# The perceptron's first products as pairs of 64 rows, with relu and window shared out, and stage 1 begun with its r chunks

## The reference

```python
h_mlp = np.maximum(pos_emb @ w1, 0.0) @ w2           # pos_emb 12480x64, w1 64x64, w2 64x128
h_filt = h_mlp * np.exp(-0.01 * pos)[:, None]
u = x * v
y = np.fft.irfft(np.fft.rfft(u, n=2*S, axis=1) * np.fft.rfft(h_filt, n=2*S, axis=0)[None], n=2*S, axis=1)[:, :S]
x1 = x * y                                           # 12480x128
x2 = np.maximum(x1 @ w_in, 0.0)**2 @ w_out           # 128 -> 2048 -> 128
h2 = x2 @ w_in2
out = (np.maximum(h2, 0.0) + alpha * np.minimum(h2, 0.0)) @ w_out2
```

## Time and profile before

| | us |
|---|---|
| median of 3 runs | 1376.6 (1376.57 to 1376.84) |
| profiled execution, its own time | 1377.39 |
| profiled execution, span of the engines' records | 1375.4 |
| TensorE busy | 1367.1 (99%) |
| VectorE busy | 1117.0 (81%) |
| ScalarE busy | 1124.1 (82%) |
| GpSimd busy | 178.9 (13%) |

### The profile page before, as it was taken

One profiled execution on the slowest core, in us unless ns is written; L12 is line 12 of the kernel. 1 busy time (PEld: TensorE's weight loads), 2 busy tenths in 40 slices (PEclk: granted clock), 3 DMA queues, 4 the chain that ended last, 5 costly groups with the idle time before them and its releaser, 6 DMA issues.

```text
span 1375.4 us, 19834 instructions
## 1 busy us (share of the span) xinstructions
PE 1367.1 (99%) x6879; PEld 1153.8 (84%) x6879; DVE 1117.0 (81%) x1398; ACT 1124.1 (82%) x1505; POOL 178.9 (13%) x200
## 2 busy tenths in 40 slices
PE   9999999999999999999999999999999999999998
PEld 8988888998888888888888888888888888888887
DVE  6888888568778877887888888887888878888888
ACT  3678888358878877888888888888888888888887
POOL 4647888410000000000000000000000000000000
PEclk9999999999999999999999999999999999999999
DMA  9648896620000100000000000000000000000000
GB/s 258 186 123 254 276 286 216 198 71 28 24 32 8 32 24 9 8 1 8 8 8 8 1 8 8 8 8 1 8 8 8 0 8 9 8 8 0 8 9 15
DMA packets 53514, 75.34 MB, mean 55 GB/s; under 512 B 5285, under 2 KB 37515, under 8 KB 53435
## 3 DMA queue, kind: packets, MB, share of 16 engines
q1 hardware_dynamic: 52507, 73.58, 17.3%
q10 hardware_dynamic: 832, 0.47, 0.1%
q0 software_dynamic: 96, 0.20, 0.1%
HBM read 54.93 MB, written 19.23 MB: 54 GB/s over the span
## 4 chain that ended last, share of the span: by engine, by line
PE 97%; ACT 1%; DVE 1%; issue 0%; DMA 0%; POOL 0%; SPq 0%; ACTq 0%; DVEq 0%; POOLq 0%
PE ps L190 13%; PE ps L192 13%; PE ps L191 13%; PE ps L205 13%; PE ps L207 13%; PE ps L206 13%; PE ps L783 5%; PE ps L820 4%; PE ps L904 3%; PE ps L798 3%; PE ps L806 2%; PE ps L791 1%; PE ps L766 1%; DVE stage L400 1%; PE ps L871 0%
## 5 line engine op out<-in xcount | busy, mean ns | idle before, releaser
L414 DVE TENSOR_TENSOR g_lo<-stage,g_hi 128x1024 fp32r<-128x1024 f32 (+2 forms) x199 | 238.2, 1198 | 164.3 <-ACT g_hi L315 163.7
L190 PE MATMUL ps<-x_hi,w_hi 128*128 128x512 f32 (+2 forms) x800 | 310.3, 388 | 0.2 <-DVE x_lo L390 0.2
L205 PE MATMUL ps<-g_hi,w_hi 128*128 128x512 f32 (+2 forms) x800 | 308.8, 386 | 0.6 <-DVE g_lo L414 0.4
L192 PE MATMUL ps<-x_lo,w_hi 128*128 128x512 f32 (+2 forms) x800 | 307.5, 384 | 0.0
L191 PE MATMUL ps<-x_hi,w_lo 128*128 128x512 f32 (+2 forms) x800 | 307.3, 384 | 0.0
L207 PE MATMUL ps<-g_lo,w_hi 128*128 128x512 f32 (+2 forms) x800 | 307.2, 384 | 0.0
L206 PE MATMUL ps<-g_hi,w_lo 128*128 128x512 f32 (+2 forms) x800 | 307.2, 384 | 0.0
L324 ACT ACTIVATE relu<-ps 128x1024 f32<-128x1024 f32 (+2 forms) x200 | 201.6, 1008 | 107.2 <-PE ps L192 104.6
L400 DVE SCALAR_TENSOR_TENSOR stage<-stage,alpha_sb 128x512 f32<-128x512 f32 (+2 forms) x400 | 276.4, 733 | 0.4 <-ACT stage L357 0.2
L357 ACT ACTIVATE stage<-ps,sign_sb 128x512 f32<-128x512 f32 (+2 forms) x400 | 251.2, 673 | 2.7 <-PE ps L192 1.4
L446 DVE TENSOR_TENSOR g_lo<-g,g_hi 128x1024 fp32r<-128x1024 f32 (+2 forms) x200 | 239.3, 1196 | 13.1 <-ACT g_hi L345 13.0
(11 more groups left out here) (68 smaller groups left out, 1213.5 us busy)
## 6 DMA issues: line engine op xcount, KB each, us to landing
g_dram<-work SPq DMA_DIRECT2D x49, 256.0 KB, 3.4
work<-dft_back SPq DMA_DIRECT2D x66, 128.0 KB, 3.6
gt<-g_dram SPq DMA_DIRECT2D x10, 784.0 KB
gt<-x_seq SPq DMA_DIRECT2D x32, 196.0 KB
work<-v_seq SPq DMA_DIRECT2D x32, 196.0 KB
work<-dft_forward SPq DMA_DIRECT2D x49, 128.0 KB, 3.5
x<-x_gate SPq DMA_DIRECT2D x16, 390.0 KB, 4.9
out_t<-x SPq DMA_DIRECT2D x23, 256.0 KB, 2.0
```

The costliest lines, as they stand in the source:

```text
L190: nc.tensor.matmul(into[:, c, :t], w_hi[k][:, at], x_hi[layer][:, :t], start=True, stop=False)
L192: last = nc.tensor.matmul(into[:, c, :t], w_hi[k][:, at], x_lo[layer][:, :t], start=False, stop=True)
L205: nc.tensor.matmul(acc[layer][:, :t], w_hi[k][:, at], hi[:, c], start=first, stop=False)
L414: nc.vector.tensor_tensor(lo[:, :, :t], g2[at][:, :, :t], hi[:, :, :t].bitcast(FP32), ALU.subtract).then_inc(g2_lo_ready, 1)
```

## The change

Three things are changed together. First, each of the 64 products becomes two of 64 rows (`HALF[half]`), one for each block, at `tile_position` (0, 0) and (64, 0), into two different banks; the moving side is one 64x64 square of w1. The weights are 128 columns of `pos_sb` instead of 98, so that 30 columns of the next residue are multiplied too, into rows of PSUM that nobody reads (the very last residue takes 98). A product therefore waits for the piece that holds the next residue. Second, of fills 1, 3 and 5 block 1 goes another way: ScalarE applies the relu and writes `h_sb`, and GpSimd multiplies this by the window, before its first x * v. Third, stage 1 begins with two r chunks, which wait for all of h, and the order of chunks is another: 16 r chunks among the first 35, then 13 u chunks. EARLY_UNITS goes from 42 to 43, EARLY_FILTER from 43 to 44.

```diff
-    order = "u" + "ruuru" * 8 + "u" * 7
+    BY_ACT = (1, 3, 5)
+    order = "rr" + "ur" * 4 + "uurur" * 5 + "u" * 13
-    EARLY_UNITS, EARLY_FILTER = units_end + 2, units_end + 3
+    EARLY_UNITS = max(units_end, place["u", U_CHUNKS - X_SLOTS] + 1) + 2
+    EARLY_FILTER = EARLY_UNITS + 1
...
     def gpsimd_program(pool):
+        pool.wait_ge(window_loaded, 16)
+        for n, i in enumerate(BY_ACT):
+            first = N1 + 8 * i
+            pool.wait_ge(h_by_act, n + 1)
+            h = h_sb[:, :, first:first + 8]
+            nc.gpsimd.tensor_tensor(h, h, window_sb[:, first:first + 8].unsqueeze(1).to_broadcast([R, HID, 8]),
+                                    ALU.mult).then_inc(h_by_pool, 1)
...
         def mlp_fill(i):
             wait(pe, h_windowed, i - 3)
+            if i - 4 in BY_ACT:
+                pe.wait_ge(h_by_act, BY_ACT.index(i - 4) + 1)
             for n in range(8):
-                if n * POS % HID == 0:
-                    pe.wait_ge(pos_loaded[(8 * i + n) * POS // HID], 16)
-                at = slice((8 * i + n) * R, (8 * i + n + 1) * R)
-                last = nc.tensor.matmul(two_banks(i % 4)[:R, n * P:(n + 1) * P], pos_sb[:, at], w1_sb,
-                                        start=True, stop=True)
+                c = 8 * i + n
+                taken = P if c < HID - 1 else R
+                pe.wait_ge(pos_loaded[min(c + 1, HID - 1) * POS // HID], 16)
+                for half in range(2):
+                    last = nc.tensor.matmul(ps[:taken, 2 * (i % 4) + half, n * HID:(n + 1) * HID],
+                                            pos_sb[HALF[half], c * R:c * R + taken], w1_sb[HALF[half], HALF[half]],
+                                            start=True, stop=True, tile_position=(N1 * half, 0))
...
         def stage1_chunk(n):
             if n < 3:
-                pe.wait_ge(h_windowed, MLP_FILLS if kind == "r" else MLP_FILLS - 3 + n)
+                pe.wait_ge(h_windowed, MLP_FILLS)
+                pe.wait_ge(h_by_pool, len(BY_ACT))
...
+    def mlp_part(i, half):
+        return ps[:R, 2 * (i % 4) + half, :].rearrange("p (n o) -> p o n", n=8), half * N1 + 8 * i
...
     def scalar_program(act):
+        for i in BY_ACT:
+            act.wait_ge(mlp_done, i + 1)
+            src, first = mlp_part(i, 1)
+            nc.scalar.activation(h_sb[:, :, first:first + 8], src, ACT.Relu).then_inc(h_by_act, 1)
...
         def window_fill(i):
-            src = two_banks(i % 4)[:R, :].rearrange("p (n h o) -> p h o n", n=8, h=2)
-            for half in range(2):
-                first = half * N1 + 8 * i
+            for half in range(1 if i in BY_ACT else 2):
+                src, first = mlp_part(i, half)
```

More of the change, by code:

```diff
@@ L570, in long_convolution @@
     mlp_done, h_windowed = sem("mlp_done"), sem("h_windowed")
+    h_by_act, h_by_pool = sem("h_by_act"), sem("h_by_pool")
     x_loaded = [sem(f"x_loaded{b}") for b in range(X_SLOTS)]
@@ L997, in window_fill @@
                 dve.wait_ge(window_loaded, 16)
-            src = two_banks(i % 4)[:R, :].rearrange("p (n h o) -> p h o n", n=8, h=2)
-            for half in range(2):
-                first = half * N1 + 8 * i
+            for half in range(1 if i in BY_ACT else 2):
+                src, first = mlp_part(i, half)
                 last = nc.vector.scalar_tensor_tensor(
-                    out=h_sb[:, :, first:first + 8], in0=src[:, half], scalar=0.0,
+                    out=h_sb[:, :, first:first + 8], in0=src, scalar=0.0,
                     in1=window_sb[:, first:first + 8].unsqueeze(1).to_broadcast([R, HID, 8]),
```

## The result

The changed kernel took 1392.54 us in the median of 21 runs, against 1376.6; the ratio is 1.0081 (95% interval 1.006 to 1.0102). It is slower, clearly by more than the 0.2% that can be told from no change, and outside the range given. The runs fall into two groups: eight between 1378.2 and 1382.2, twelve between 1392.0 and 1394.1. Before shows no such groups (21 runs within 1.2 us). Each run also has a mean granted clock over its span, with the time ahead of the first recorded change of level put at 1.00. In the lower group it is 1.000 in the quickest run (1378.19 us), 0.997 in the slowest (1382.16) and 0.999 in the other six. In the upper group it is 1.000 or 0.999 in nine runs and 0.989 in three.

A forecast was written before the change was run, and what follows sets the result against it. TensorE was taken to bound the kernel, so savings at the start reach the end. Start -1.85, first gap -0.2, tables +0.5, ScalarE's copies +0.1 make -1.45 us: median 1376.6 to 1375.1, range 1373.6 to 1378.7.

The forecast's parts named there:

- The pair's price: L766's products: a pair of 64-row products takes 60 ns, so a fill takes 1 us against 1.75.
- The upper bound: Most that a new pair of L766 could take: 0.11 us, read from L806, which has such pairs already.
- The argument against it: First two loads lie 0.11 to 0.12 us apart at both clock levels, so this is a burst's start, not the rate.
- A late rise would be made up behind the landings: At the start, a late rise of TensorE's clock costs nothing, since landings of pos_t pace the fills.
- The clock's rival: TensorE's clock falls before stage 1, two r chunks cost +2.7 us: about 1377.8; chance 0.07.
- What paces the fills: Perceptron fills: landings of pos_t pieces, 1.2 us for a fill's two, set the pace; last fill ends at 15.75.
- Window, relu, GpSimd: During fills: VectorE's half 0.65 us, ScalarE's relu some 0.6, GpSimd's product 1.27; the third ends at 14.8, before x*v.
- if the cover were gone: Start of stage 1: GpSimd's window products could then put up to 3.8 us in front of the first x*v.
- Beginning with r: Start of stage 1: TensorE idles from 15.7 to 17.2 for h; first chunk at 17.2 against 19.02, -1.85 us.
- the loads' rival: L766: loads at 0.108 us set the pace, fills end as now, stage 1 starts 1.4 us later; 1378.4 us, chance 0.27.
- The new order of chunks: Stage 1: as many short stalls as before, no difference; only the first gap of 0.2 us goes.
- The end of stage 1: dft_forward tables land late behind x and v before unit_spectra(0): +0.5 us taken, 1 at worst, nothing at best.

The follow-up runs named there:

- e6: e2 with 14 warm-up products instead of 7, so that the higher clock level comes before the pairs; 1378.05 us, ratio 1.001.
- e5: e2 with 128 moving columns instead of 64 in seven products of eight (h of block 1 ends as zeros); 1376.91 us, ratio 1.0007.
- e1: The changed kernel again, no edit; 1392.16 us, ratio 1.0083.
- e2: The changed kernel's pairs of 64 rows alone: VectorE does all windows, chunk order and early places as before the change; 1391.72 us, ratio 1.0112.
- e7: The changed kernel with 98 columns of weights in all products and the old waits for pos_t; 1377.03 us, ratio 1.0024.
- e8: e4 with 98 columns of weights and 98 moving, block 1 in reverse order within a fill, waiting for both pieces at its start; 1375.18 us, ratio 0.9991.
- e4: The changed kernel with stage 1 in the old chunk order and EARLY_UNITS 42; 1390.26 us, ratio 1.0064.
- e9: e8 with VectorE doing all windows and relus (BY_ACT empty); 1375.77 us, ratio 0.9996.
- e11: e8 with the changed kernel's order of stage 1 (r chunks first, EARLY_UNITS 43); 1376.33 us, ratio 1.0.
- e12: e8 with two fills (1 and 3) partly on ScalarE and GpSimd instead of three; 1375.77 us, ratio 0.9994.
- e3: The kernel before the change with only the new chunk order, its EARLY_UNITS and stage 1 waits; 1378.86 us, ratio 1.0016.
- e10: e3 with unit_spectra(0) and filter_spectra(0) one chunk later; 1377.58 us, ratio 1.0006.

## Why the prediction was wrong

**The pair's price: the step that failed.** The prediction put a pair at 60 ns between bounds of 53 and 110. With 128 columns of weights it is 0.11 us at the higher level, with 64 moving columns (e6) and with 128 (e5), and 0.213 at the lower (e1, e2). With 98 columns of weights it is 0.087 at the higher level (e7), and 0.17 at the lower (e8, ten pairs in 1.69 us; there the moving side has 98 columns too, so this figure fits but does not tell the two apart). That is two cycles of TensorE's clock for each column of weights and a few ns: 128 columns are 107 ns at 2.4 GHz and 213 at 1.2, 98 are 82 and 163. The upper bound was the answer, and the nearest row, L806, had the number, though with 128 moving columns it could not show the cause. The 0.11 us between the first two loads at the higher level was the rate. The argument against it leaned on one gap of 0.12 us at the lower level (the first two loads of all, 98 columns), shorter than the 0.163 that these columns take in a stream there; that one gap was no measure of a stream.

The Trainium skill's rule ("TensorE: Matmul & The Clock Gate", "LDWEIGHTS (loading the stationary operand)") would have given the right fill at the higher level, 107 ns for 128 columns. It gives no other figure for the low clock; here the measurement decides: at the lower level 128 columns took 0.213 us. With 107 ns at both levels the low clock would do the loads no harm, and the 14 us would have been missed.

**"A late rise would be made up behind the landings": the second step that failed, and the dearer one.** The clock's rival was named, but at the wrong place (a fall before stage 1) and with too small a price. That fall did happen, in the first profile, for 3.4 us. But the upper group, as its three traces show it, is a rise that does not come while pairs run. Nothing is made up, since loading is the bound and follows the clock: 3.41 us a fill against landings of 1.2 us. In a pair of 64 moving columns, the moving side has nothing to do for half of the time that the loads take. That this half-empty moving side is what keeps the level low is shown from two sides. With 128 moving columns instead of 64, and the same rows, loads and waits, none of 11 runs stays low (e5). With the higher level reached before the first pair, none of 11 falls into the group (e6). Without either, 4 of 4 (e2), 8 of 12 (e4), 7 of 11 (e1) and 12 of 21 runs are in it. Between them stands e7, 64 moving columns to 98 of weights, with 3 of 12; and where both are 98 (e8, e9, e11, e12) it is 0 of 44.

Two reservations. e5 and e6 ran on another chip than e1, e2 and e4, and e2 itself never ran there; against the chip as the cause, e7 ran on the chip of e5 and e6 and has an upper group. And what puts one run of the same kernel into the one group and the next into the other stays open. In the lower group's profile the level rose near 4.8 us, when five pairs had run behind the warm-up; in e2's it had not risen by then, and no pair brought it.

**What paces the fills.** The prediction let the landings of pos_t set the pace; in the changed kernel the loads did, and one wait of 0.24 us is all that its trace puts down to a piece. It came to more only with quicker pairs: 0.99 us in e7, 1.56 in e8, which waits for two pieces at once. The landings themselves were near what was read (piece 4 after 5.4 us, 5.6 before).

**Window, relu, GpSimd.** Sizes right. Two things followed from slow fills: with 1.79 us a fill VectorE needed no help, and GpSimd's third product came so late (16.44) that it held up the first x*v, the case that the prediction priced only "if the cover were gone".

**Beginning with r.** Priced at 1.4 us of idle time for TensorE; 1.44 measured (1.47 in e3). With the last fill where it was, nothing paid for it: 20.68, the 20.5 of the loads' rival.

**The new order of chunks.** No difference by itself beyond that: right, as far as e3 shows.

**The end of stage 1.** +0.5 was taken, 1 at worst. The wait was 0.77 us, and the whole loss about 0.9 to 1.2: e10 gave 1.3 us back by one chunk. The cause was right, the size was near the upper bound.

**The sum.** The loads' rival said 1378.4; the lower group's runs are at 1378.2 to 1382.2. The one at 1378.19 has no fall of the clock on record and is at that sum; the seven above it all have one (a mean below 1.000). e3 with e10 and e4's lower runs confirm its parts one by one. A chance of 0.27 for that rival and 0.07 for the clock were both too small, and none was given to the two coming together.

## What to carry to other kernels

- Splitting a product into row groups pays only where moving columns set the pace. Here a load of fp32 weights takes as long per column as moving one (107 ns for 128 of either), so a pair that moves fewer columns than it loads is no quicker than its load, and every column of weights taken beyond need is paid (128 for 98: 0.11 for 0.087 us).
- Look at what the change does to how densely TensorE's moving side is filled where the clock has not yet risen. A start that is only half filled can hold the lower level until dense work comes (here till 37 us), and then everything of TensorE's in it takes twice as long; compare several runs, since one profile may show the mild case.
- Work moved ahead of another engine's queue (GpSimd's windows, tables behind x and v) should be priced with the arrival times of the slow case too.

## What the runs showed of the hardware

- The higher level, once reached, was kept by half-filled pairs for 14 us (e6 and the first profile), while the same pairs did not bring it up in 27 us (e1, e2, e4). So the level hangs on what was done before. That pairs always keep it is not shown: the nine runs with a mean of 0.989 or 0.990 speak against it.
- The clock fell for 3.4 us behind 1.44 us of idle time in the first profile, and behind 1.56 us in e8's; behind 1.47 us after full products (e3) it fell in none of 11 runs (e10: two of 11 have a mean of 0.999).
- One of 21 runs took 5749.84 us. No trace of it exists; it stays open.
- Columns that a product writes too many can be written over by the next for nothing (e8): filling the moving side up to the load's length cost no time.
